# Attention in front of a token mix: score tiles in groups of four and three, one bank each, with the key sums between two halves of the value products

## The reference

```
scores = cap * tanh((q @ k.T / 8) / cap);  attn = exp(scores) / sum(exp(scores))
x = attn @ v                                            # 48 heads
theta = x @ w_theta
y = w_tok_r @ (x cos theta) + w_tok_i @ (x sin theta);  u = x + y
u = u + relu(u @ w_ch)
u = u + (relu(u.T @ w_tok1) @ w_tok2).T                 # token block
out = u + relu(u @ w_ch1) @ w_ch2                       # channel block
```

## Time and profile before

| what | value |
|---|---|
| median of 3 runs | 938.94 us |
| the profiled execution: its time, its span | 940.34 us, 938.5 us |
| PE, DVE, ACT, POOL busy | 896.8, 444.0, 307.2, 215.8 us |
| mean granted clock of the PE | 0.989 |
| first score product | 7.35 us |
| first angle product | 205.02 us |
| first product of the token mix | 236.76 us |

### The profile page before, as it was taken

The page is one execution under the profiler, slowest core; times in us unless marked ns, Lnnn a source line. Parts: engine busy times, 40 slices in busy tenths (PEclk is TensorE's granted clock), DMA queues, the critical chain, the costliest instruction groups (busy, mean ns, idle before and its releaser), DMA issues.

```text
span 938.5 us, 12749 instructions
## 1 busy us (share of the span) xinstructions
PE 896.8 (96%) x5248; PEld 756.9 (81%) x5248; DVE 444.0 (47%) x625; ACT 307.2 (33%) x370; POOL 215.8 (23%) x187
## 2 busy tenths in 40 slices
PE   7888888879999999999999999999999999999998
PEld 5444444449899989999999999999999999999997
DVE  4788888768857594953443434322301030021102
ACT  5888888835324232532120212211100100010000
POOL 2354656424414151426000004800000000000000
PEclk8999999989999999999999999999999999999999
DMA  6344555330202010320000014700300030001001
GB/s 187 100 120 125 153 147 149 99 107 11 59 1 68 1 59 1 102 84 23 1 1 0 1 59 156 239 1 1 117 1 1 1 117 0 0 0 59 1 1 59
DMA packets 41955, 56.60 MB, mean 60 GB/s; under 512 B 7280, under 2 KB 38064, under 8 KB 41904
## 3 DMA queue, kind: packets, MB, share of 16 engines
q1 hardware_dynamic: 41904, 55.88, 19.7%
HBM read 41.45 MB, written 8.34 MB: 53 GB/s over the span
## 4 chain that ended last, share of the span: by engine, by line
PE 84%; ACT 6%; DVE 5%; issue 3%; DMA 1%; POOL 0%; SPq 0%; DVEq 0%; ACTq 0%; POOLq 0%
PE psum L1023 24%; PE psum L1024 24%; PE psum L1025 24%; ACT ring L622 6%; PE psum L1069 5%; PE psum L1037 5%; PE psum L1082 2%; PE psum L1175 1%; DVE sin_z L875 1%; DVE reduced L868 0%; PE psum L1126 0%; ACT ring L625 0%; DVE reduced L864 0%; DVE tile_sums L781 0%; DMA kq_raw<-kq_t 0%
## 5 line engine op out<-in xcount | busy, mean ns | idle before, releaser
L1007 DVE SCALAR_TENSOR_TENSOR relu_lo<-psum,relu_hi 128x448 fp32r<-128x448 f32 x48 | 30.0, 625 | 281.0 <-PE psum L1025 264.1
L744 ACT ACTIVATE relu_hi<-psum 128x448 fp32r<-128x448 f32 x48 | 26.2, 546 | 312.7 <-PE psum L1025 303.0
L1024 PE MATMUL psum<-relu_lo,mlp 128*128 128x448 f32 x288 | 106.1, 368 | 0.0
L1025 PE MATMUL psum<-relu_hi,mlp 128*128 128x448 f32 x288 | 106.1, 368 | 0.0
L1025 PE MATMUL psum<-u_hi,mlp 128*128 128x448 f32 x288 | 106.1, 368 | 0.0
L1023 PE MATMUL psum<-relu_hi,mlp 128*128 128x448 f32 x288 | 106.1, 368 | 0.0
L1024 PE MATMUL psum<-u_lo,mlp 128*128 128x448 f32 x288 | 106.1, 368 | 0.0
L1023 PE MATMUL psum<-u_hi,mlp 128*128 128x448 f32 x288 | 106.0, 368 | 0.0
L622 ACT ACTIVATE ring<-psum,score_scale 128x1344 f32<-128x1344 f32 x56 | 76.8, 1371 | 29.3 <-PE psum L1037 27.8
L625 ACT ACTIVATE ring<-ring,cap_col 128x1344 f32<-128x1344 f32 x56 | 79.5, 1419 | 1.8
L1069 PE MATMUL psum<-ring,values 128*32 128x448 f32 x768 | 76.6, 539 | 0.0
(11 more groups left out here) (133 smaller groups left out, 2065.1 us busy)
## 6 DMA issues: line engine op xcount, KB each, us to landing
kq_raw<-kq_t SPq DMA_DIRECT2D x48, 224.0 KB, 3.8
mlp_raw<-moe_w_ch SPq DMA_DIRECT2D x24, 384.0 KB, 6.7
values<-v SPq DMA_DIRECT2D x24, 224.0 KB, 2.6
inverse_rows<-sum_scratch SPq DMA_DIRECT2D x48, 112.0 KB, 3.4
x_batch<-x_t SPq DMA_DIRECT2D x4, 1344.0 KB, 6.5
out_t<-x_t SPq DMA_DIRECT2D x8, 672.0 KB, 3.2
u_scratch<-x_t SPq DMA_DIRECT2D x2, 1344.0 KB, 5.3
x_t<-u_scratch SPq DMA_DIRECT2D x2, 1344.0 KB, 6.1
```

Source lines behind the costliest of these rows:

```text
L744: act.activation(relu_hi[c % 3][:, :], psum[:, c % 2, 0:SEQ], ACT.Relu).then_inc(relu_hi_made, 1)
L1007: dve.scalar_tensor_tensor(out=relu_lo[c % 3][:, :], in0=psum[:, c % 2, 0:SEQ], scalar=0.0, in1=relu_hi[c % 3][:, :].bitcast(F32), op0=ALU ...
L1024: pe.matmul(out, left[0], right[1], start=False, stop=False)
L1025: return pe.matmul(out, left[1], right[0], start=False, stop=stop)
```

## The change

- **Banks and groups.** Tile i of a pair uses bank i, in the order A0, A1, B0, B1, A2, T, B2; group 0 is the first four, group 1 the last three, in every pair. The value products use bank 7, the key sums bank 3, which is B1's. The ring holds two pairs.
- **Order on the PE.** Score slots are (A0, B0), (A1, B1), (A2, T), (T, B2); T is opened in the third and closed in the fourth. Per pair: scores of p+1, value products of group 0 (`weigh_first`), key sums of p-1, value products of group 1 (`weigh_second`). The key sums wait for the tanh on group 0 of pair p+1, whose bank they use.
- **Sums by fours.** Each pair's sums are stored to DRAM alone; once in four pairs they are loaded into 64 partitions, inverted, stored and spread in two DMAs of four pairs each, with one buffer.
- **Values.** The masked tiles come from the DMA: the values are loaded in two halves of the partitions, and the empty halves are set to zero once, in three buffers. `pad_values` is gone.
- **POOL.** Token weights are split in three pieces (1344, 1344, 448 elements), theirs and theta's loads are spread over the turns of SP; POOL scales four pairs in a row and makes x_hi of batch 0 after pair 11. The scaling of the last four pairs stands behind the lo parts of the first three tiles of the mix.
- **Start.** The second DMA of pair 0 and that of cap go through the ACT's queue, and an extra tanh on one column stands ahead of everything.
- **Seam.** The DVE makes x_lo of batch 0 before pair 22, the key sums of pair 23 stand behind the first tile of angles.

```diff
-GROUP = 3
-N_GROUPS = N_PAIRS * PAIR_TILES // GROUP
-RING_PAIRS = 3
-RING_GROUPS = RING_PAIRS * PAIR_TILES // GROUP
-A0, A1, B0, T, B1, A2, B2 = range(PAIR_TILES)
+RING_PAIRS = 2
+A0, A1, B0, B1, A2, T, B2 = range(PAIR_TILES)
+GROUPS = ((0, 4), (4, PAIR_TILES))
+VALUES_BANK, SUMS_BANK = 7, 3
+BATCH_OF_SUMS = 4
+N_SUMS = N_PAIRS // BATCH_OF_SUMS
...
+                if pair + 2 < N_PAIRS:
+                    after(sp, values_summed, pair)
+                    load_v(sp, pair + 2)
+                if pair % 4 == 1 and pair > 4:
+                    load_sums(pair // 4 - 1)
+                if pair % 4 == 3 and pair > 4:
+                    spread_inverses(pair // 4 - 1)
+                if pair in (1, 3):
+                    load_token(pair // 2)
+                if pair == 4:
+                    load_token(2)
+                for chunk, turn in enumerate((4, 8, 10, 12, 14, 16)):
+                    if pair == turn:
+                        load_theta(chunk)
+                if pair == N_PAIRS - 3:
                     sp.wait_ge(heads_scaled, 2 * D_TILES)
                     copy_x(0)
-                if pair + 2 < N_PAIRS:
-                    sp.wait_ge(values_padded, pair + 1)
-                    sp.wait_ge(values_summed, pair + 1)
-                    load_v(sp, pair + 2)
-            spread_inverses(N_PAIRS - 3)
-            store_inverses(N_PAIRS - 2)
-            gather_sums(N_PAIRS - 1)
-            spread_inverses(N_PAIRS - 2)
-            store_inverses(N_PAIRS - 1)
-            spread_inverses(N_PAIRS - 1)
+                if pair % 4 == 2 and pair > 4:
+                    store_inverses(pair // 4 - 1)
+                if pair >= 1:
+                    store_sums(pair - 1)
...
+            for piece in range(3):
+                split_token(piece)
+            for chunk in range(2):
+                split_theta(chunk)
+            for batch in range(2):
+                for pair in range(BATCH_OF_SUMS * batch, BATCH_OF_SUMS * (batch + 1)):
+                    scale_heads(pair)
+                for chunk in range(2 * batch + 2, 2 * batch + 4):
+                    split_theta(chunk)
+            for pair in range(2 * BATCH_OF_SUMS, 2 * D_TILES):
+                scale_heads(pair)
+            pool.wait_ge(heads_scaled, 2 * D_TILES)
+            x_b = x_tile(0, 0, D_TILES).rearrange("p (d n) -> p d n", n=SEQ)
+            next_b = x_tile(1, 0, D_TILES).rearrange("p (d n) -> p d n", n=SEQ)
+            pool.tensor_copy(x_hi[:, :, 0:SEQ], x_b).then_inc(x_hi_made, 1)
+            pool.tensor_copy(x_hi[:, :, SEQ:XW], next_b[:, :, SEQ - TAIL:SEQ]).then_inc(x_hi_made, 1)
+            for pair in range(2 * D_TILES, N_PAIRS - BATCH_OF_SUMS):
                 scale_heads(pair)
 
             for b in range(BATCH):
                 for m, (half, t) in enumerate(ANGLE_TILES[b]):
                     n = BEFORE[b] + m
+                    if n == 3:
+                        for pair in range(N_PAIRS - BATCH_OF_SUMS, N_PAIRS):
...
+            load_keys_second(act, 0)
+            act.dma_start(cap_col[:, :], cap.partition_broadcast(P)).then_inc(cap_loaded, 16)
+            act.wait_ge(consts_made, 1)
+            act.activation(warm[:, :], half_pi[:, :], ACT.Tanh)
             act.wait_ge(scale_made, 2)
-            act.wait_ge(consts_made, 1)
-            for group in range(N_GROUPS):
-                first = GROUP * (group % RING_GROUPS)
-                places = ring[:, first:first + GROUP, :]
-                banks = slice(GROUP * (group % 2), GROUP * (group % 2) + GROUP)
-                act.wait_ge(scores_ready, group + 1)
-                if group >= RING_GROUPS:
-                    act.wait_ge(keys_summed, (GROUP * (group - RING_GROUPS) + GROUP - 1) // PAIR_TILES + 1)
-                act.activation(places, psum[:, banks, 0:SEQ], ACT.Tanh, scale=score_scale[:, :]
-                               ).then_inc(tanh_done, 1)
-                act.wait_ge(tanh_done, group + 1)
-                act.activation(places, places, ACT.Exp, scale=cap_col[:, :]).then_inc(probs_ready, 1)
+            for pair in range(N_PAIRS):
+                for group, (first, end) in enumerate(GROUPS):
+                    places = ring[:, ring_place(pair, first):ring_place(pair, end - 1) + 1, :]
+                    act.wait_ge(scores_ready, group_end(pair, group))
+                    if pair >= RING_PAIRS and group == 0:
+                        act.wait_ge(values_summed, pair - RING_PAIRS + 1)
+                        act.wait_ge(tiles_added, pair - RING_PAIRS + 1)
+                    elif pair >= RING_PAIRS:
+                        act.wait_ge(keys_summed, pair - RING_PAIRS + 1)
+                    act.activation(places, psum[:, first:end, 0:SEQ], ACT.Tanh, scale=score_scale[:, :]
+                                   ).then_inc(tanh_done, 1)
+                    act.wait_ge(tanh_done, group_end(pair, group))
+                    act.activation(places, places, ACT.Exp, scale=cap_col[:, :]).then_inc(probs_ready, 1)
...
-            for pair in range(N_PAIRS - 1):
-                if pair + 2 < N_PAIRS:
-                    split_kq(pair + 2)
-                if pair >= 2:
-                    invert(pair - 2)
+            def attention(pair):
+                if pair % 4 == 2 and pair > 4:
+                    invert(pair // 4 - 1)
+                add_first(pair)
                 if pair >= 1:
                     copy_sums(pair - 1)
-                add_tiles(pair)
+                add_second(pair)
                 copy_heads(pair)
+
+            for pair in range(N_PAIRS - 2):
+                split_kq(pair + 2)
+                attention(pair)
...
-            invert(N_PAIRS - 3)
-            dve.wait_ge(scores_ready, N_GROUPS)
-            x_b = x_tile(0, 0, D_TILES).rearrange("p (d n) -> p d n", n=SEQ)
-            next_b = x_tile(1, 0, D_TILES).rearrange("p (d n) -> p d n", n=SEQ)
-            dve.wait_ge(heads_scaled, 2 * D_TILES)
-            dve.tensor_copy(x_hi[:, :, 0:SEQ], x_b).then_inc(x_hi_made, 1)
-            dve.tensor_copy(x_hi[:, :, SEQ:XW], next_b[:, :, SEQ - TAIL:SEQ]).then_inc(x_hi_made, 1)
+            dve.wait_ge(mix_weights_split, 9)
             make_x_lo(0)
-            copy_sums(N_PAIRS - 2)
-            add_tiles(N_PAIRS - 1)
-            copy_heads(N_PAIRS - 1)
-            copy_sums(N_PAIRS - 1)
-            invert(N_PAIRS - 2)
+            for pair in range(N_PAIRS - 2, N_PAIRS):
+                attention(pair)
...
+            def score_slot(pair, n, a_tile, a_block, b_tile, b_block):
 
                 s = pair % 2
                 a_rows, b_rows = slice(0, HEAD_DIM), slice(HEAD_DIM, P)
+                a_keys, b_keys = [slice(block * P, (block + 1) * P) for block in (a_block, b_block)]
                 queries = slice(BANK, KQ)
+                for step, (left, right) in enumerate(((kq_hi, kq_hi), (kq_hi, kq_lo), (kq_lo, kq_hi))):
+                    b_mm = pe.matmul(psum[:, b_tile, 0:SEQ], left[s][b_rows, b_keys],
+                                     right[s][b_rows, queries], start=step == 0,
+                                     stop=step == 2 and b_tile != T)
+                    if step == 0 and a_tile == T:
+                        pe.wait_ge(tail_opened, pair + 1)
+                    a_mm = pe.matmul(psum[:, a_tile, 0:SEQ], left[s][a_rows, a_keys],
+                                     right[s][a_rows, queries], start=step == 0 and a_tile != T,
+                                     stop=step == 2)
+                if b_tile == T:
+                    b_mm.then_inc(tail_opened, 1)
+                if n % 2 == 1:
+                    a_mm.then_inc(scores_ready, 1)
 
             def score(pair):
 
                 pe.wait_ge(kq_split, pair + 1)
+                after(pe, tanh_done, group_end(pair - 1, 0))
+                score_slot(pair, 0, A0, 0, B0, 1)
+                after(pe, sums_copied, pair - 2)
+                score_slot(pair, 1, A1, 1, B1, 2)
+                after(pe, tanh_done, group_end(pair - 1, 1))
+                score_slot(pair, 2, A2, 2, T, 0)
+                score_slot(pair, 3, T, 3, B2, 3)
+
+            def weigh_slot(pair, n, a_values, a_tile, b_values, b_tile):
+
+                own = values[pair % VALUE_BUFFERS]
+                for j, (block, tile) in enumerate(((a_values, a_tile), (b_values, b_tile))):
+                    for h in range(2):
+                        rows = slice(HEAD_DIM * j + 32 * h, HEAD_DIM * j + 32 * h + 32)
+                        mm = pe.matmul(psum[rows, VALUES_BANK, 0:SEQ], own[:, block, 32 * h:32 * h + 32],
+                                       ring[:, ring_place(pair, tile), :], start=n == 0, stop=n == 3)
+                return mm
+
+            def weigh_first(pair):
+
+                pe.wait_ge(v_loaded[pair % VALUE_BUFFERS], 32 * (pair // VALUE_BUFFERS + 1))
                 after(pe, heads_copied, pair)
+                pe.wait_ge(probs_ready, group_end(pair, 0))
+                weigh_slot(pair, 0, V_A, A0, V_B, B0)
```

(35 more changed lines are left out.)

293 lines of the change are left out of this document (120 added, 173 removed).

## The result

The changed kernel takes **913.8 us** (median of 4 runs, 912.9 to 915.5) beside 939.3 for the kernel before (938.8 to 940.1, 4 runs): a ratio of 0.973, 95% interval 0.971 to 0.975. Forecast were 906 and a range of 899 to 920. The profiled execution took 912.9, its span 910.9; before, 940.3 and 938.5. So the span fell by 27.6 us, where the prediction's sum had 34.1. The 6.5 between them are what the experiments had to find.

What follows compares the result with a forecast made beforehand. A loop passing between three nearly full engines, with tanh waiting for score products, bounded the kernel. A 6.75 us period, earlier start and seam put the mix 34.1 us earlier: 940.3 - 34.1 = 906.2, forecast 906, range 899 to 920.

Steps and rivals of the forecast that it cites:

- rival (a): Attention pairs: VectorE, lengthened by POOL's work, becomes the bound; +9 us, kernel at 915; chance 20%.
- a period of 6.7 to 6.8: Middle of attention: 6.7 to 6.8 us between one four-tile tanh and the next, named as a sign.
- a mix less than 30 behind the angles: Seam after attention: mix starts less than 30 us after the angles' start, named as a sign; 29.0 forecast.
- tail wait: TensorE, fourth score slot: closing T waits for its opening one slot before; 0.22 us a pair, bounds 0 to 0.31.
- Both loops close within 0.1 us of each other: Attention pair: TensorE's loop, 6.75 us, and the tanh loop, next score half ending at 6.75 + 0.2, nearly equal.
- Rival (b): Attention: TensorE's new wait costs nothing, ScalarE bounds at 6.37 us a pair; kernel at 899; chance 13%.
- (c): First pairs: granted clock falls for longer, two more pairs at 1.2 GHz; kernel at 919; chance 7%.
- (d): Attention: VectorE and POOL exclude each other wholly, 8.7 us a pair; kernel at 945; chance 3%.
- (e): Attention: something else of the reordering holds, the bank shared by B1 and key sums making a longer loop; chance 2%.
- the cover: Attention: VectorE's results are due 1.4 us or more after it gives them, covering one blocked instruction at a time.
- the 2.6 worked out by it: POOL's rounding of x, by the exclusive-lock rule: four microseconds less the 1.4 of cover, +2.6 in the sum.
- a tile costs it 3.3: Angles at the seam: each tile costs VectorE 3.3 us, more with POOL beside it; mix starts right behind the angles.

Runs made afterwards that it cites:

- T apart: Changed kernel with score slots reordered to (A0,B0), (A2,T), (A1,B1), (T,B2), so one slot lies between opening and closing T: 910.8 us, 0.969.
- paddings: Changed kernel with two 32-column POOL multiplications a pair put back, into a scratch tile: 913.9 us, 0.973; with T's opening and closing one slot apart as well, 910.6 us.

## Why the prediction was right, and where its sum was off

The direction, the cause and the stated range held. The forecast's own range of 901 to 911 didn't: 913.8 lies beside rival (a)'s 915, though not for its reason. Of the signs that the prediction named, two failed, a period of 6.7 to 6.8 (6.88) and a mix less than 30 behind the angles (32.05).

**Period: right in its mechanism, the tail wait mis-sized.** "Both loops close within 0.1 us of each other", with 6.53 of products and 0.22 of new wait. Measured 6.57 (T apart) and 0.31, the upper of the two bounds. I had taken a value near the 0.20 that the 0.40 of latency gave, and left out the 0.11 of refilling behind the wait, which the other bound had in it. That is 0.09 a pair; the other 0.04 lie in the products (6.57 for 6.53). Together 0.13 x 20 = 2.6 us.

**ScalarE and VectorE: right.** ScalarE's work is 6.43 (forecast 6.3), its wait for the key sums 0.45 (0.2). Rival (a), VectorE as the bound, is out: paddings cost nothing in the medians and at most some 2 us, and the quiet pairs have no wait for VectorE. Rival (b) is out by the same 6.43 and by the tail wait of 0.31, (c) by a granted clock of 1.00 from 22 us on, (d) and (e) by a period of 6.88.

**POOL's rounding: the cover failed.** Taken as 4 us, it took 2.42, and still cost 1.85 where the sum had nothing. "Which covers one blocked instruction at a time" was the failing step: scaling, inversion and rounding came in one pair, and the kq_lo subtract (1.98 for 1.16), the inversion's product (1.16 for 0.20) and the add were held one after the other, which used up the 1.4 of cover before the rounding came. The Trainium skill (SBUF — State Buffer, "Who interferes with whom") says that who issues second waits for the whole instruction; the pieces in place of one rounding agree (add 2.91 against 1.04), and the 2.6 worked out by it in the prediction stand nearer to 1.85 than the sum's zero. That nearness is in part luck: the 2.6 priced a rounding of 4 us, and with the measured 2.42 the same working gives 2.42 - 1.4 = 1.0.

**Start.** First tanh at 8.82 for 8.3: the second half of kq(0) in ScalarE's queue brought 0.1 of the 0.6. The clock stood at 0.61 from 14 to 18 us, 1.6 us for the 2 taken. Value products of pair 21 ended at 166.57, for 161.8: 0.5 + 2.6 + 1.85, less 0.2 that is left over (0.4 less for the clock, 0.3 more in the pair of 7.18, and smaller ones).

**Seam: right to the angles, wrong to the mix.** From pair 21 to the angles 11.8 (forecast 11.9). Then "a tile costs it 3.3 ... that should let the mix start right behind the angles": 32.05 where I took 29.0 and an upper bound of 31.7. The failing step is the 3.3 for a tile. It was read from one tile (221.76 in the earlier trace rows) beside which POOL had nothing to do. The view that groups the line shows, in the trace of before, that this tile was the exception:

```profile
L875 DVE TENSOR_SCALAR sin_z<-reduced x28: 347/1162/1175, 213.0 to 395.1; 128x384 f32<-128x384 f32 x28
```

A median of 1162 ns beside a minimum of 347: over half of these steps stood behind POOL, and such a tile costs 4.76 in the changed kernel. The Trainium skill (SBUF — State Buffer, "Who interferes with whom") says that a VectorE instruction with both inputs in SBUF contends with a reading GpSimd one, and one with at most one SBUF input and outside the two-port modes doesn't; here 1.26 for 0.56, and 0.54 to 0.56 for each product with a PSUM operand, agree. The last step (L897) has one input, in SBUF, and was held as well, 1.16 for 0.35; by that rule it would have to run in a two-port mode, which no run here shows. Moving the inverse rows early, as the change does, puts POOL's scaling (5.31 for four) on top.

Sum: 0.5 + 2.6 + 1.85 - 0.2 - 0.1 + 3.05 = 7.7 late at the mix, and 1.2 back behind it: 6.5. I had put this last term at nothing. The clock stood at 0.71 from 236 to 241 us before and stands at 1.00 from 210 to 215 now, and the first and the third mix take 0.6 less each (27.30 before, 26.71 after for the first).

## What to carry to other kernels

Before a cost is taken from one row, look at the minimum and median of its group: where they are far apart, two regimes are mixed, and the one that the change will meet has to be priced. What a helper engine costs goes by the length of its single instructions rather than by its busy time: one of 2.42 us held the critical engine's chain, and 48 short ones cost next to nothing; so cut the long ones, or move them beside work whose second operand lies in PSUM. When a loop is brought under a new bound, the delays that the old one hid come up, so that a gain per turn must not be multiplied by the number of turns before one has looked for them.

## What the hardware did that I had not expected

- A product that opens a bank for the other rows of the array costs its neighbour 0.31 us when it stands in the slot right ahead, and nothing that shows with one slot between (a score part of 2.62 for 2.98).
- TensorE idling 1.85 of some 9 us in each pair had its granted clock at 0.83 on the mean for 50 us. The kernel before, whose TensorE was busy 43.55 of 50 us where this one was busy 41.81, kept 1.00, and its stands for the tanh were 0.9 at the longest. What of the two makes the difference the runs don't show.
- VectorE's 64x56 product takes 0.20 alone and 1.16 behind one POOL instruction: held 0.96, a small instruction loses as much as a large one (kq_lo's subtract in the same pair lost 0.82).
- Six roundings of 448 columns on POOL take 5.22, one of 2688 takes 2.42. Part of the 5.22 is POOL standing behind VectorE in its turn (a piece takes 0.56 at its shortest, 1.42 at its longest). Cutting a POOL instruction raises its busy time and still gains, where another engine waits behind it.
